# Moving one VectorE subtraction within the attention stage of an attention, MLP and soft-mixture kernel

## The reference

```python
# q, k, v: (4, 8, 1152, 64)
q_pool = q.reshape(B, H, S // 2, 2, D).mean(axis=3)
scores = scale * np.matmul(q_pool, k.transpose(0, 1, 3, 2))
scores = scores - np.max(scores, axis=-1, keepdims=True)
attn = np.exp(scores)
attn = attn / (np.sum(attn, axis=-1, keepdims=True) + 1e-09)
x = np.matmul(attn, v)                    # then heads side by side: (2304, 512)
h = x @ w_in                              # (2304, 2048)
g = np.where(h > 0.0, h, np.exp(np.minimum(h, 0.0)) - 1.0)
x = g @ w_out
...                                       # soft mixture: 8 experts, 4 slots each
```

## Time and profile before

| what | us |
|---|---|
| median of 3 runs | 949.84 |
| lowest and highest | 949.2, 951.02 |
| profiled execution | 950.26 |
| its span, first to last instruction | 948.4 |
| PE busy in the span | 900.7 |
| DVE busy | 566.8 |
| POOL busy | 387.5 |

### The profile page before, as it was taken

One profiled execution on the slowest core, in us unless ns is written; L12 is line 12 of the kernel. 1 busy time (PEld: TensorE's weight loads), 2 busy tenths in 40 slices (PEclk: granted clock), 3 DMA queues, 4 the chain that ended last, 5 costly groups with the idle time before them and its releaser, 6 DMA issues.

```text
span 948.4 us, 18067 instructions
## 1 busy us (share of the span) xinstructions
PE 900.7 (95%) x7120; PEld 729.7 (77%) x7120; DVE 566.8 (60%) x966; ACT 387.9 (41%) x740; POOL 387.5 (41%) x269
## 2 busy tenths in 40 slices
PE   4899999999999999998999999999999999999995
PEld 3666666666666666665799999999999999999733
DVE  6888877888787778776465433433433443443323
ACT  3555555555555556446343322322322322322202
POOL 3999888888888888888200000000000000000000
PEclk9999999999999999999999999999999999999999
DMA  6112212221121122202240000200000000377898
GB/s 236 51 52 76 63 39 76 76 76 65 62 76 37 65 76 76 93 2 84 72 136 1 1 1 1 89 1 1 2 1 1 1 1 1 109 243 224 281 383 291
DMA packets 47027, 76.41 MB, mean 81 GB/s; under 512 B 3296, under 2 KB 32608, under 8 KB 46944
## 3 DMA queue, kind: packets, MB, share of 16 engines
q1 hardware_dynamic: 46944, 75.26, 23.8%
HBM read 70.53 MB, written 4.72 MB: 79 GB/s over the span
## 4 chain that ended last, share of the span: by engine, by line
PE 48%; POOL 2%; SPq 1%; DMA 1%; issue 0%; DVE 0%; ACT 0%; POOLq 0%; ACTq 0%; DVEq 0%
PE psum L678 7%; PE psum L660 7%; PE psum L680 7%; PE psum L662 7%; PE psum L679 7%; PE psum L661 7%; POOL acc L1499 2%; PE psum L798 1%; SPq L467 1%; DMA ring<-in_w 1%; PE psum L716 1%; PE psum L698 1%; PE psum L722 1%; PE psum L609 0%; PE psum L703 0%
## 5 line engine op out<-in xcount | busy, mean ns | idle before, releaser
L1499 POOL TENSOR_TENSOR acc<-acc,pt 128x576 f32<-128x576 f32 x220 | 329.2, 1496 | 48.2 <-ACT pt L935 21.0
L935 ACT ACTIVATE pt<-psum 128x576 f32<-128x576 f32 x288 | 174.1, 649 | 138.3 <-PE psum L596 137.8
L1141 DVE TENSOR_REDUCE mx<-psum 128x1 f32<-128x512 f32 x256 | 162.0, 676 | 9.8 <-PE psum L531 7.5
L609 PE MATMUL psum<-pt,vs 128*64 128x288 f32 x1152 | 153.6, 411 | 0.0
L1330 DVE TENSOR_SCALAR gf<-gf 128x384 f32<-128x384 f32 x96 | 34.5, 360 | 196.8 <-ACT gf L1064 196.8
L678 PE MATMUL psum<-gh,W 128*128 128x384 f32 x384 | 133.4, 347 | 0.0
L1064 ACT ACTIVATE gf<-psum 128x384 f32<-128x384 f32 x96 | 47.2, 492 | 200.7 <-PE psum L662 200.1
L679 PE MATMUL psum<-gl,W 128*128 128x384 f32 x384 | 128.5, 335 | 0.0
L680 PE MATMUL psum<-gh,W 128*128 128x384 f32 x384 | 128.4, 334 | 0.0
L662 PE MATMUL psum<-xh,W 128*128 128x384 f32 x384 | 128.4, 334 | 0.0
L660 PE MATMUL psum<-xh,W 128*128 128x384 f32 x384 | 128.4, 334 | 0.0
(11 more groups left out here) (163 smaller groups left out, 1826.0 us busy)
## 6 DMA issues: line engine op xcount, KB each, us to landing
ring<-in_w SPq DMA_DIRECT2D x16, 1024.0 KB, 5.3
ring<-in_w SPq DMA_DIRECT2D x32, 512.0 KB, 7.7
qraw<-in_qT SPq DMA_DIRECT2D x16, 576.0 KB, 4.8
kraw<-in_kT SPq DMA_DIRECT2D x16, 576.0 KB, 3.7
vs<-in_v SPq DMA_DIRECT2D x16, 576.0 KB, 3.9
out<-ob SPq DMA_DIRECT2D x18, 256.0 KB, 4.0
wst<-in_w_in SPq DMA_DIRECT2D x16, 256.0 KB, 2.8
wst<-in_w_out SPq DMA_DIRECT2D x16, 256.0 KB, 3.4
```

The source lines that it names most:

```text
L609: ins = mm(psum[64 * s:64 * s + 64, O_BANK, 0:HALF], vs[:, p % NB, s, kt * D:(kt + 1) * D], pt[:, i % NPT, s, :], start=(kt == 0), stop=(k ...
L935: act.activation(pt[:, i % NPT, :, :], t_pair(("T", h, kt))[:, :, 0:HALF], ACT.Exp, scale=SCALE)\
L1141: dve.tensor_reduce(mx[:, b, u // 2, s, u % 2:u % 2 + 1], bank, AX.X, ALU.max).then_inc(s_red, 1)
L1499: pool.tensor_tensor(a, first, pt[:, i % NPT, :, :], ALU.add).then_inc(s_acc, 1)
```

## The change

The call of `queries_lo(p + 1)` goes from the end of even halves to their middle, to stand right behind the second `keys_lo` of the same pair and ahead of the late unit's reductions. Its condition stays the same, so does the number of calls, 14. Nothing else is touched.

```diff
                     if h and h % 2 == 0 and p + 1 < NP:
                         keys_lo(p + 1, 1)
+                        queries_lo(p + 1)
                     reduce_items(s_items(h, LATE))
                     if h:
                         reciprocals(h - 1, 0)
...
             reduce_items(s_items(h, END))
-            if h and h % 2 == 0 and p + 1 < NP:
-                queries_lo(p + 1)
             if h == 0:
                 queries(2)
```

## The result

| | before | changed |
|---|---|---|
| median us | 950.23 | 936.34 |
| lowest and highest | 949.2, 951.02 | 935.84, 938.16 |
| span of the profiled execution | 948.4 | 934.4 |
| first matmul of the MLP (L660), us from the start of the span | 463.4 | 450.8 |

The ratio of the times is 0.9858, with an interval of 0.9841 to 0.9875: 13.9 us less, where 12.7 were forecast. (The median of before holds a fourth execution here; the forecast of 937.1 us started from 949.84, the median of three.) The attention stage ends 12.6 us earlier.

What follows compares the result with a forecast made beforehand. TensorE, busy 95% of the span, was taken as the bound. Removed waits of 14.2 us less 1.5 us lateness gave 12.7 us, so the profiled 950.26 became 937.6 and the median forecast 937.1 us; range 934.0 to 945.8, holding 0.84.

Steps and rivals of the forecast that it cites:

- The place of the wait: Odd half's second score unit: PE waits because q's subtraction delays normalizing and the bank-freeing reduction; 14 waits, 14.9 us.
- What is late next: Odd half after the change: normalizing waits for the products of V, 0.19 us after the first unit's start.
- The gain in odd halves: Second unit of odd halves starts 1.09 to 1.18 us earlier; 14.2 us gained in all.
- The prediction's 0.05 us: Odd halves: part of each removed PE wait given back later in the half, 0.05 us off each of 14.
- The port: Middle of even halves: VectorE and POOL take turns; q's subtraction ends 0.61 us after an add ends.
- The lateness: Diagonal unit's reduction in even halves starts late: 0.04 us in 12 pairs, 0.5 in two early ones; 1.5 us.
- The bound of 0.73: Diagonal reduction in even halves: at most 0.73 us late, if an add has just begun when k's subtraction is issued.
- No reserve behind the diagonal unit: Even half from the diagonal reduction to the last unit: each 0.1 us late costs PE 0.1 us.
- POOL: Attention stage: POOL's waits for exponentials, 1.8 us per pair, of which 1.0 would go, so POOL does not become the bound.
- the port does not take most of it in all pairs: Denies rival 1: unfavourable POOL turn in all pairs, 10.2 us late, 4.0 us gain left, 945.8 us; chance 0.12.
- no two adds pass before q's subtraction: Denies rival 2: two adds behind k's subtraction, diagonal reduction 1.61 us late, 8.4 us lost, 958.2 us; chance 0.07.
- no new wait stands on PE in the regular part: Denies rival 3: the wait returns under another name, POOL's, a pair stays at 27.3 us, 949.8 us; chance 0.06.

Runs made afterwards that it cites:

- e2: Changed kernel plus one unused one-operand VectorE reduction at the end of the 14 even halves, where q's subtraction stood; 939.11 us, ratio 0.9891.
- e3: Changed kernel plus two unused one-operand VectorE reductions at the end of the 14 even halves; 948.79 us, ratio 0.999.
- e5: Changed kernel with POOL's adds at key tiles 2, 3 and 4 of even halves (all but the last) cut to one column; 935.39 us, one execution.
- e7: The changed kernel itself, unedited, run again on the same chip as a kernel with q's subtraction in odd halves; 936.73 us, ratio 0.9857.
- e1: Changed kernel with q's subtraction one step further down, behind the late (diagonal) unit's two reductions; 946.5 us, ratio 0.9968.
- e4: Changed kernel with q's subtraction moved to the middle of odd halves, behind the first part of k for the same pair; 937.55 us, ratio 0.9867.
- e6: Changed kernel with q's subtraction in the middle of odd halves, run again beside the changed kernel on one chip; 936.96 us, ratio 0.9862.

## Why the prediction was right, point by point

- **The place of the wait.** Right: it was the subtraction in front of normalizing. e2 and e3 bring it back with another instruction in the same place; a first 0.46 us are free there, and the second instruction costs its full length. The prediction read a turn of POOL in this subtraction too, but it did not say that half of its 1.50 us is the wait for that turn.
- **What is late next.** Right: the products of V. Normalizing came at the first unit's start plus 0.18 us (0.19 said).
- **The gain in odd halves.** 14.2 us forecast. 14 x (5.14 - 4.14) = 14.0 measured, first unit to products. The second unit itself moved by 2.62 - 1.46 = 1.16 us per pair (1.09 to 1.18 said), and 0.17 us of it were given back by the products. The prediction's 0.05 us were taken off the waits (1.06 us a pair), which are shorter than the way by which the unit moved, and off those they are right: 1.00 us was won. In the expectation of e2 I took the same 0.05 off the full way, where 0.17 belong; that is 0.12 of the 0.2 us a pair by which it was too high.
- **The port.** Right: turns of one add each, 0.61 us from an add's end to the subtraction's end. No subtraction for q had its turn ahead of the add, and none had to let two pass. e5 shows the cause.
- **The lateness.** 1.5 us forecast, 14 x 0.09 = 1.2 measured, and made up much as forecast: about 0.04 us in each of the regular pairs, and 0.68 in one early pair where two of 0.5 each were put. Which early pair meets an add that has just begun was not foreseen; the pair at 78 us of before, on which this was founded, grew by 0.01 us. The pair at 187 us: the reduction began 0.60 us behind the diagonal matmul (186.45 to 187.05), before the change 0.54 (217.62 to 218.16), so 0.06 late where 0.04 was said. The bound of 0.73 was nearly reached once: the third of the even halves has 13.87 us, 0.68 more than before the change (13.88 in e7), and PE's new wait of 0.54 us. There k's subtraction came as an add had just begun:

```profile
104.27 1.40 POOL L1498 TENSOR_TENSOR acc<-acc,pt 128x576 f32<-128x576 f32 x1
...
104.29 2.00 DVE L1206 TENSOR_TENSOR klr<-kraw,khr 128x576 fp32r<-128x576 f32 x1
106.21 1.97 DVE L1211 TENSOR_TENSOR qlr<-qs,qhr 128x576 fp32r<-128x576 f32 x1
```

- **No reserve behind the diagonal unit.** Right by e1: 0.75 us there cost 0.66 us of the even half in 13 of 14 pairs.
- **POOL.** Right: it still waits 9.1 us for exponentials from 60 to 411 us, 0.7 us per pair (0.8 said).
- **The sum.** For the attention stage 12.7 us forecast, 12.6 measured. The time fell by 13.9. The remaining 1.4 us of the span lie behind 463.4 and 450.8 us, and their cause stays open. PE waited there once for a load of weights (L821), 1.4 us before and 0.2 after; but e4 has that wait of 1.4 us too, and its part from the first L660 to the end is 483.0 us. That part is 485.0 us before, 483.6 in the changed kernel, 484.2 in e7, which is the same kernel, and 482.6 in e6, so it varies by as much from run to run. It is also longest in the three kernels with the longest attention stage (before, e1 and e3, 484.7 to 485.0 us), so that a part of it may hang on the change is not excluded. The forecast has no term for it, and I don't count it as the change's.

The rivals fell thus: the port does not take most of it in all pairs, but in one; no two adds pass before q's subtraction; and no new wait stands on PE in the regular part, but for the 0.54 us in that one pair. The prediction had named a new wait as a sign of being wrong; this one stands in one of 14 pairs and is inside the bound of 0.73 us that it had worked out.

## What to carry to other kernels

When an in-order engine feeds a bank ring, look not at its busy share but at what stands ahead of each instruction that frees a bank, and move free work to where the engine waits for the bottleneck anyway. Count the reserve of each place: here 2 us fitted ahead of the diagonal unit, while 0.75 us one step behind it cost 0.66. Give a moved instruction the length that it has in its new neighbourhood, not its mean.

## What the runs showed that was not expected

The same subtraction, 576 columns with two SBUF operands, took 0.75, 1.50 or 1.95 us by its place: 0.75 beside a pausing POOL (e5, and 13 of 14 in e1), 1.5 as the median before, and 1.95 to 1.97 in each of the 14 cases behind another one. VectorE never kept its turn though its next instruction started 0.07 us before the former ended. The other surprise is how little the first 0.66 us at the end of an even half cost in e2: 0.20 us. The third is how much one late reduction can cost: in e1 a wait of 1.64 us was followed by 3.3 us at half the clock.
